# Two weight sums of the first dense unit move within GpSimd's queue, past a key decay and a query decay

## The chip, the cores and the metric

The kernel runs on one core of a Trainium2 chip. The metric is the device time of one execution in microseconds. Of the kernel before there are three timed runs, 581.52, 581.63 and 581.82 us.

## The reference, cut to what matters

```python
# q, k, v: batch 2, heads 8, sequence 768, head size 64, float32
state = gamma * state + outer(k[t], v[t])          # one 64x64 state for each batch and head
y[t]  = scale * q[t] @ state                       # decaying linear attention
x = y as (1536, 512)
h = x @ w_in;  x = (h * sigmoid(1.702 * h)) @ w_out          # dense layer 1, 512 -> 2048 -> 512
xn = x / rms(x) * rms_g
x = (silu(xn @ w_gate) * (xn @ w_val)) @ w_out               # dense layer 2, 512 -> 1536 -> 512
```

## The kernel before

**Attention.** The sequence of each of the 2 batches is cut into 6 chunks of 128 tokens: 12 chunks a = 0 to 11, where 0 to 5 are the first batch. Each engine has one queue, in the order in which its program is written, and works through the chunks in passes of two (`for a in range(0, STEPS, 2)`). For a chunk TensorE does the scores (L396), the products of decayed keys and values that are added to the state ("new products", L413), the part of the output that comes from the state ("from state", L428) and the part from the chunk itself ("from chunk", L441). VectorE masks the scores (L891) and copies or decays the state out of PSUM ("new state", L903 and L906). GpSimd multiplies the keys by their decay ("key decay", `decay_k`, L1039) and, from chunk 7 on, the queries by theirs ("query decay", `decay_q`, L1047). Chunks 5 and 11, the last of each batch, need no key decay and no new products; chunks 0 and 6 need no query decay. ScalarE copies the outputs to SBUF (L694).

In a pass a TensorE's order is: scores of both chunks, from state of both, new products of a + 1, from chunk of both, new products of a + 2. A chunk's new products wait for its key decay and for the new state of the step before; its from-state product waits for its query decay and the same state.

**The first dense unit.** The dense layers multiply blocks in the scheme of Strassen and Winograd, with seven products in place of eight, and each float32 operand is split in a high and a low half that TensorE reads as fp32r. A unit of weights is one transfer to `raw`. GpSimd makes four sums of its blocks (`weight_sum(r, k)`, k = 0 to 3, at L1054, L1057, L1060 and L1064), ScalarE makes the high halves (L605) and VectorE the low halves (L773). In the same way x is summed by VectorE (L795, L796, L799, L803), and split by ScalarE (L624) and VectorE (L782). The sums and splits of unit 0 and of the first batch's x are written between the attention passes, so that TensorE can go from the last from-chunk product straight to the first dense product (L479 to L482). SyncE issues the transfer of unit 0's weights at 16.39 us, behind the key and value transfers of chunks 5 and 6.

VectorE's order around the change, with the chunk or block in brackets: masked (4, 5), low half x (B11, B21), new state (6; the table names it by the chunk that it takes in), masked (6, 7), new state (7), x sums at L795 and L796, low half of weights L773, new state (8), masked (8, 9), low half x (T1), new state (9), low half x (B22), low half of weights, new state (10), masked (10, 11), and the remaining sums and halves.

**GpSimd's order**, by passes, before:

| pass a | order in the queue |
|---|---|
| 2 | key decay 3, key decay 4 |
| 4 | weight sum 0, key decay 6, weight sum 1 |
| 6 | query decay 7, key decay 7, weight sum 2, key decay 8, weight sum 3 |
| 8 | query decays 8 and 9, key decays 9 and 10 |
| 10 | query decays 10 and 11 |

Weight sum 0 waits for the transfer of `raw`; sum 1 waits for sum 0, sum 2 for sum 1, sum 3 for sum 0.

Of the kernel before, what the change touches and what calls it, by code (L numbers as in the profile page):

```python
# [61 lines left out]
def transformer_kernel(nc, attn_in, tables, ident_in, gain_in, w1, w2, out):  # L62
    with ExitStack() as ctx:
# [112 lines left out]
        for p, (layer, _) in enumerate(PHASES):  # L176
            units += [("hidden", p, j) for j in range(HIDDEN[layer])]
            units += [("project", p, j) for j in range(PROJECT[layer])]
# [74 lines left out]
        def cols(i, size):  # L253
            return slice(i * size, i * size + size)
# [39 lines left out]
        def state_at(a):  # L294

            g, c = chunk_of(a)
            return (CHUNKS - 1) * g + min(c, CHUNKS - 1)

        def cross_at(a):

            g, c = chunk_of(a)
            return (CHUNKS - 1) * g + max(c - 1, 0)
# [6 lines left out]
        def set_growth(engine, c):  # L309
            for h in range(HEADS):  # L310
                ins = engine.memset(k_growth[:, HEADS * c + h:HEADS * c + h + 1], HEAD_DIM ** 0.5 * gamma(h) ** (-CHUNK * c))
            return ins
# [70 lines left out]
        def _(pe):  # L383
# [202 lines left out]
            for p, (layer, _) in enumerate(PHASES):  # L586
                for j in range(HIDDEN[layer]):
                    hidden(p, j)
                    if p in (1, 2) and j == 4:
                        norm_totals(p - 1)  # L590
                    if p in (1, 2) and j == 6:
                        norm_bcast(p - 1)
                project_phase(p)

        @block.scalar
        def _(act):
# [117 lines left out]


            for p, (layer, _) in enumerate(PHASES):
                for j in range(HIDDEN[layer]):
                    n, r = h_at[p, j], at["hidden", p, j]
# [307 lines left out]
        @block.gpsimd  # L1026
        def _(pool):
            for c in range(LEAVES):
                ins = set_growth(pool, c)
            ins.then_inc(factors_set, 1)  # L1030
            pool.memset(minus_half[:, :], -0.5).then_inc(half_set, 1)

            def decay_k(a):
                r, m = a % SLOTS, state_at(a)
                pool.wait_ge(kv_in[r], 16 * (a // SLOTS) + 16)
                if m >= 2:
                    pool.wait_ge(kv_done, m - 1)
                k, kd = (t.rearrange("p (h d) -> p h d", h=HEADS) for t in (slot[r][:, 1024:1536], k_dec[m % 2]))
                pool.tensor_tensor(kd, k, k_table[:, cols(a % CHUNKS, HEADS)].unsqueeze(2).to_broadcast([P, HEADS, HEAD_DIM]),  # L1039
                                   ALU.mult).then_inc(k_decayed, 1)  # L1040

            def decay_q(a):
                r, x = a % SLOTS, cross_at(a)
                pool.wait_ge(qk_in[r], 16 * (a // SLOTS) + 16)
                if x >= 2:
                    pool.wait_ge(cross_done, x - 1)
                pool.tensor_tensor(q_dec[x % 2], slot[r][:, 0:512], q_table, ALU.mult)\  # L1047
                    .then_inc(q_decayed[1], 1)

            def weight_sum(r, k):  # L1050
                s1, a11, a12, a21, a22, s2, s4 = (raw[r % 2][:, cols(k, 256)] for k in range(7))
                if k == 0:
                    pool.wait_ge(raw_in[r % 2], 16 * (r // 2) + 16)
                    pool.tensor_tensor(s1, a21, a22, ALU.add).then_inc(w_sums, 1)  # L1054
                elif k == 1:
                    pool.wait_ge(w_sums, sums_at[r] + 1)
                    pool.tensor_tensor(s2, s1, a11, ALU.subtract).then_inc(w_sums, 1)  # L1057
                elif k == 2:
                    pool.wait_ge(w_sums, sums_at[r] + 2)
                    pool.tensor_tensor(s4, a12, s2, ALU.subtract).then_inc(w_sums, 1)  # L1060
                else:

                    pool.wait_ge(w_sums, sums_at[r] + 1)
                    pool.tensor_tensor(a21, a11, a21, ALU.subtract).then_inc(w_sums, 1)  # L1064

            pool.wait_ge(k_table_set, 1)
            decay_k(0)
            for a in range(0, STEPS, 2):
                for b in (a, a + 1):
                    if b > CHUNKS:  # L1070
                        decay_q(b)
                if (a + 1) % CHUNKS < CHUNKS - 1:
                    decay_k(a + 1)
                if a in (4, 6):
                    weight_sum(0, a - 4)
                if a + 2 < STEPS:
                    decay_k(a + 2)
                if a in (4, 6):
                    weight_sum(0, a - 3)

            for r, (kind, p, j) in enumerate(units):
                if kind == "hidden":
                    if r == 1:

                        pool.wait_ge(x_lo_done, 6)
                    for k in range(4):
                        if r > 0:
                            weight_sum(r, k)
                    if p in (1, 2) and j == 6:
                        pool.wait_ge(half_set, 1)  # L1090
                        pool.wait_ge(mean_done, p)
                        pool.tensor_tensor(inv_rms[:, :], mean_sq[:, :], minus_half[:, :], ALU.pow)\
                            .then_inc(inv_done, 1)
# [56 lines left out]
```

## Time and profile before

| | us |
|---|---|
| median of three runs | 581.63 |
| profiled execution, own time | 581.93 |
| its span | 580.1 |
| TensorE busy | 572.4 (99%) |
| VectorE busy | 360.9 (62%) |
| ScalarE busy | 297.8 (51%) |
| GpSimd busy | 170.4 (29%) |

The span is the part of the execution that the profile shows, from its first instruction to its last. The execution's own time is 1.83 us more. An engine's busy time counts its instructions alone; what it waits for stands as idle time before the next instruction. In the rows below PE is TensorE, DVE VectorE, ACT ScalarE and POOL GpSimd. The slot buffers, the decayed keys and queries, the state and the masked scores all lie in one tensor and have the name `arena`.

### The profile page before, as it was taken

Reading aid. Unit: us, or ns where it says so; the run is one execution under the profiler, and the core shown is the slowest. Engines: PE = TensorE matmul, PEld = TensorE weight load, DVE = VectorE, ACT = ScalarE, POOL = GpSimd, SP = SyncE. Lnnn points to the kernel's source line nnn. Section 1 sums busy time; section 2 is a strip of 40 time slices with the busy share of each in tenths; the row PEclk is TensorE's granted clock in tenths of the full one; section 3 lists DMA queues with packets and bytes.
Section 4 is the critical chain, followed back from the end, with each engine's and each line's share of the span. In section 5 each row is a group of like instructions: output and inputs, shape, how many; then the busy total and the mean of one; then the engine's idle time right before and its main releaser. Section 6 shows DMA issues by size and latency. Waiting matters only on the chain.

```text
span 580.1 us, 9395 instructions
## 1 busy us (share of the span) xinstructions
PE 572.4 (99%) x3638; PEld 551.0 (95%) x3638; DVE 360.9 (62%) x486; ACT 297.8 (51%) x501; POOL 170.4 (29%) x222
## 2 busy tenths in 40 slices
PE   7999999999999999999999999999999999999997
PEld 7989999999999999999999999998889999998886
DVE  5899555666325667776336778668755666666432
ACT  1244766654326767544237655574435555564321
POOL 2395643000223461000315454400051545420000
PEclk8999999999999999999999999999999999999999
DMA  8971222322102222312202222232214222224202
GB/s 319 403 284 37 74 72 73 110 72 75 52 21 73 73 72 74 110 41 68 73 0 76 72 73 73 74 101 82 74 36 139 79 73 73 73 74 115 67 1 108
DMA packets 24220, 52.84 MB, mean 91 GB/s; under 512 B 1776, under 2 KB 1904, under 8 KB 24176
## 3 DMA queue, kind: packets, MB, share of 16 engines
q1 hardware_dynamic: 23312, 49.36, 25.6%
q10 hardware_dynamic: 864, 2.88, 1.3%
q8 instruction: 29, 0.48, 0.3%
q14 instruction: 15, 0.12, 0.1%
HBM read 49.09 MB, written 3.15 MB: 90 GB/s over the span
## 4 chain that ended last, share of the span: by engine, by line
PE 93%; DMA 3%; issue 2%; POOL 1%; ACTq 0%; DVE 0%; POOLq 0%
PE bank L532 20%; PE twin L532 20%; PE twin L479 11%; PE twin L482 11%; PE twin L481 11%; PE bank L482 6%; PE bank L481 6%; PE bank L479 6%; DMA arena<-attn_in 3%; PE bank L441 1%; PE bank L428 1%; PE bank L573 0%; POOL arena L1047 0%; PE twin L396 0%; ACTq L684 0%
## 5 line engine op out<-in xcount | busy, mean ns | idle before, releaser
L773 DVE TENSOR_TENSOR w_lo<-raw,w_hi 128x512 fp32r<-128x512 f32 (+2 forms) x148 | 148.9, 1022 | 49.9 <-ACT w_hi L605 49.5
L1054 POOL TENSOR_TENSOR raw<-raw 128x256 f32<-128x256 f32 x40 | 31.4, 786 | 323.3 <-DMA raw<-w 316.5
L479 PE MATMUL twin<-x_hi,w_hi 128*128 128x384 f32 x360 | 120.6, 335 | 0.0
L482 PE MATMUL twin<-x_hi,w_lo 128*128 128x384 f32 x360 | 120.3, 334 | 0.0
L481 PE MATMUL twin<-x_lo,w_hi 128*128 128x384 f32 x360 | 120.3, 334 | 0.0
L605 ACT ACTIVATE w_hi<-raw 128x512 fp32r<-128x512 f32 (+2 forms) x148 | 109.0, 762 | 19.7 <-PE bank L532 7.6
L808 DVE TENSOR_TENSOR g_lo<-arena,g_hi 128x768 fp32r<-128x768 f32 x56 | 54.5, 973 | 75.2 <-ACT g_hi L635 75.2
L635 ACT ACTIVATE g_hi<-arena 128x768 fp32r<-128x768 f32 x56 | 47.4, 847 | 103.8 <-PE bank L532 103.8
L479 PEld LDWEIGHTS twin<-x_hi,w_hi 128*128 128x128 f32 x360 | 67.6, 188 | 0.2 <-issue 0.2
L481 PEld LDWEIGHTS twin<-x_lo,w_hi 128*128 128x128 f32 x360 | 67.6, 188 | 0.0
L482 PEld LDWEIGHTS twin<-x_hi,w_lo 128*128 128x128 f32 x360 | 67.6, 188 | 0.0
L479 PE MATMUL bank<-x_hi,w_hi 128*128 128x384 f32 x200 | 66.9, 334 | 0.0
L481 PE MATMUL bank<-x_lo,w_hi 128*128 128x384 f32 x200 | 66.8, 334 | 0.0
L482 PE MATMUL bank<-x_hi,w_lo 128*128 128x384 f32 x200 | 66.8, 334 | 0.0
L1064 POOL TENSOR_TENSOR raw<-raw 128x256 f32<-128x256 f32 x40 | 45.4, 1136 | 0.0
L532 PE MATMUL twin<-g_hi,w_hi 128*128 128x384 f32 x128 | 42.8, 334 | 0.0
L532 PE MATMUL twin<-g_lo,w_hi 128*128 128x384 f32 x128 | 42.8, 334 | 0.0
L532 PE MATMUL twin<-g_hi,w_lo 128*128 128x384 f32 x128 | 42.8, 334 | 0.0
L532 PE MATMUL bank<-g_lo,w_hi 128*128 128x384 f32 x128 | 42.8, 334 | 0.0
L532 PE MATMUL bank<-g_hi,w_hi 128*128 128x384 f32 x128 | 42.8, 334 | 0.0
L532 PE MATMUL bank<-g_hi,w_lo 128*128 128x384 f32 x128 | 42.8, 334 | 0.0
L1060 POOL TENSOR_TENSOR raw<-raw 128x256 f32<-128x256 f32 x40 | 38.0, 951 | 3.1
(99 smaller groups left out, 997.8 us busy)
## 6 DMA issues: line engine op xcount, KB each, us to landing
raw<-w SPq DMA_DIRECT2D x68, 512.0 KB, 3.4
arena<-attn_in SPq DMA_DIRECT2D x20, 512.0 KB, 9.0
arena<-attn_in ACTq DMA_DIRECT2D x4, 512.0 KB, 12.7
out<-x SPq DMA_DIRECT2D x1, 1536.0 KB, 8.6
out<-x SPq DMA_DIRECT2D x6, 256.0 KB, 2.0
arena<-tables ACTq DMA_DIRECT2D x1, 512.0 KB, 6.1
arena<-tables ACTq DMA_DIRECT2D x1, 256.0 KB, 9.8
ident<-ident_in SPq DMA_DIRECT2D x1, 64.0 KB, 8.5
```

Source lines behind the costliest of these rows:

```text
L428: mm = pe.matmul(gate[par][rows, cols(p, P)], state[x % 2][rows, cols(p, 64)], q_dec[x % 2][rows, cols(p, P)], start=p == 0, stop=False, s ...
L479: pe.matmul(dst, w_hi[q][:, w], x_hi[:, x], start=start and kk == 0, stop=False, skip_group_check=True)
L481: pe.matmul(dst, w_hi[q][:, w], x_lo[:, x], start=False, stop=False, skip_group_check=True)
L482: mm = pe.matmul(dst, w_lo[q][:, w], x_hi[:, x], start=False, stop=kk == 1, skip_group_check=True)
L532: mm = pe.matmul(dst, a, x, start=f == 0 and k == 0, stop=f == TILES[layer] - 1 and k == 2, skip_group_check=True)
L605: act.activation(w_hi[q % 3][:, dst], src, ACT.Copy).then_inc(w_hi_done, 1)
L635: act.activation(g_hi[ft % 3][:, :], g32[:, cols(f, SEQ)], ACT.Copy).then_inc(g_hi_done, 1)
L773: dve.tensor_tensor(w_lo[q % 3][:, dst], src, w_hi[q % 3][:, dst].bitcast(F32), ALU.subtract)\
L808: dve.tensor_tensor(g_lo[ft % 3][:, :], g32[:, cols(f, SEQ)], g_hi[ft % 3][:, :].bitcast(F32), ALU.subtract).then_inc(g_lo_done, 1)
L1054: pool.tensor_tensor(s1, a21, a22, ALU.add).then_inc(w_sums, 1)
L1060: pool.tensor_tensor(s4, a12, s2, ALU.subtract).then_inc(w_sums, 1)
L1064: pool.tensor_tensor(a21, a11, a21, ALU.subtract).then_inc(w_sums, 1)
```

## The change

The order of GpSimd's queue in passes 2 to 6. The number of instructions, their operands and their waits stay as they are, and no other engine's program is touched. After the change pass 2 is key decay 3, key decay 4, weight sum 0, weight sum 1; pass 4 is key decay 6, weight sum 2, weight sum 3; pass 6 is query decay 7, key decay 7, key decay 8. As one line:

```
before: k4 | w0 k6 w1 | q7 k7 w2 k8 w3 | q8 q9 k9 k10 | q10 q11
after:  k4 w0 w1 | k6 w2 w3 | q7 k7 k8 | q8 q9 k9 k10 | q10 q11
```

```diff
                 if (a + 1) % CHUNKS < CHUNKS - 1:
                     decay_k(a + 1)
-                if a in (4, 6):
-                    weight_sum(0, a - 4)
                 if a + 2 < STEPS:
                     decay_k(a + 2)
-                if a in (4, 6):
-                    weight_sum(0, a - 3)
+                if a in (2, 4):
+                    weight_sum(0, a - 2)
+                    weight_sum(0, a - 1)
```

## Rows read from the trace of the kernel before

**Rows 1.** The page's busy times and shares of the span, with instructions.
```profile
PE 572.4 (99%) x3638; PEld 551.0 (95%) x3638; DVE 360.9 (62%) x486; ACT 297.8 (51%) x501; POOL 170.4 (29%) x222
```

**Rows 2.** Windows: length; busy of PE, PEld, DVE, ACT, POOL; PEclk, DMA, GB/s.
```profile
50.10:570.00 519.90, 519.90 (x2885) 504.03 (x2884) 319.47 (x412) 282.62 (x478) 144.28 (x158) 1.00 0.22 71
```

**Rows 3.** Timeline of PE: start, length, instructions, idle before them and its releaser.
```profile
25.44 1.96 PE L428 MATMUL bank<-arena 64*64 64x128 f32 x32
...
29.41 0.69 PE L413 MATMUL bank<-arena 128*64 128x64 f32 x16
...
33.18 0.69 PE L413 MATMUL bank<-arena 128*64 128x64 f32 x16
...
38.05 1.09 PE L428 MATMUL bank<-arena 64*64 64x128 f32 x16
40.00 1.09 PE L428 MATMUL bank<-arena 64*64 64x128 f32 x16 [0.86 <-POOL arena L1047]
...
41.54 1.92 PE L441 MATMUL bank<-arena 128*64 128x128 f32 x32
43.28 0.63 PE L413 MATMUL bank<-arena 128*64 128x64 f32 x16
...
45.83 2.08 PE L428 MATMUL bank<-arena 64*64 64x128 f32 x32
47.86 2.32 PE L441 MATMUL bank<-arena 128*64 128x128 f32 x32
```

**Rows 4.** Timeline of POOL around the four weight sums.
```profile
26.82 0.72 POOL L1054 TENSOR_TENSOR raw<-raw 128x256 f32<-128x256 f32 x1 [5.93 <-DMA raw<-w]
27.50 1.76 POOL L1039 TENSOR_TENSOR arena<-arena 128x512 f32<-128x512 f32 x1
29.22 1.44 POOL L1057 TENSOR_TENSOR raw<-raw 128x256 f32<-128x256 f32 x1
30.63 1.27 POOL L1047 TENSOR_TENSOR arena<-arena 128x512 f32<-128x512 f32 x1
...
33.56 1.03 POOL L1039 TENSOR_TENSOR arena<-arena 128x512 f32<-128x512 f32 x1
34.56 1.44 POOL L1064 TENSOR_TENSOR raw<-raw 128x256 f32<-128x256 f32 x1
35.96 3.94 POOL L1047 TENSOR_TENSOR arena<-arena 128x512 f32<-128x512 f32 x2
39.86 2.04 POOL L1039 TENSOR_TENSOR arena<-arena 128x512 f32<-128x512 f32 x2
```

**Rows 5.** Timeline of DVE in the same stretch.
```profile
26.94 3.14 DVE L782 TENSOR_TENSOR x_lo<-x,x_hi 128x768 fp32r<-128x768 f32 x2
...
31.23 2.36 DVE L891 TENSOR_TENSOR arena<-twin,arena 128x1024 f32<-128x1024 f32 x2 [0.68 <-PE twin L396]
33.91 0.42 DVE L906 TENSOR_TENSOR arena<-bank,arena 128x256 f32<-128x256 f32 x1 [0.33 <-PE bank L413]
34.25 1.16 DVE L795 TENSOR_TENSOR t<-x 128x768 f32<-128x768 f32 x1
35.33 1.48 DVE L796 TENSOR_TENSOR x<-x 128x768 f32<-128x768 f32 x1
36.74 2.03 DVE L773 TENSOR_TENSOR w_lo<-raw,w_hi 128x768 fp32r<-128x768 f32 x1
38.69 0.41 DVE L906 TENSOR_TENSOR arena<-bank,arena 128x256 f32<-128x256 f32 x1
39.02 2.34 DVE L891 TENSOR_TENSOR arena<-twin,arena 128x1024 f32<-128x1024 f32 x2
41.28 1.43 DVE L782 TENSOR_TENSOR x_lo<-x,x_hi 128x768 fp32r<-128x768 f32 x1
42.64 0.41 DVE L906 TENSOR_TENSOR arena<-bank,arena 128x256 f32<-128x256 f32 x1
```

**Rows 6.** Key and value transfer of chunk 9, issued at 28.47: issue to landing.
```profile
DMA to landing us min/median/max: 7.4/7.4/7.4
```

## The prediction

> **What bounds the kernel now.** I read the page's busy times first: TensorE is busy 99% of the span [rows 1]. The windows then say where it has room: from 50.10 to 570.00 it is busy for all of 519.90 us [rows 2]. So there is no slack behind the attention stage, and whatever moves the first dense product (50.11) moves the end by as much. Before that point the timelines of three engines have to be laid side by side.
>
> TensorE [rows 3] has one named wait behind the weights' arrival: from state of chunk 9 starts at 40.00 after 0.86 us idle, released by GpSimd's query decay. A smaller one has no label: new products of chunk 6 start at 29.41, and key decay 6 ends at 27.50 + 1.76 = 29.26 [rows 4], so they follow it at 0.15 us. GpSimd [rows 4] waits 5.93 us for the weights until 26.82 and has no idle time from there to the end of its query decays. VectorE [rows 5] waits 0.33 us for TensorE at 33.91 (new state 7), and from there each of its rows starts where the one before ends. So from 33.91 on VectorE too passes a delay on.
>
> **How GpSimd and VectorE meet.** Rows 4 and 5, side by side, show a pattern. When both have an instruction whose two inputs are in SBUF, the recorded ends alternate at fixed distances: key decay 8 ends at 34.59, the sum at L795 at 35.41, weight sum 3 at 36.00, the sum at L796 at 36.81, and, past the first query decay, the low half at L773 at 38.77 and query decay 9 at 39.90. The held-up VectorE instruction of 768 elements ends 0.82 after GpSimd's, a held-up weight sum 0.59 after VectorE's, a held-up query decay 1.13 after. At the start the same: weight sum 0 ends at 27.54, so the first L782 at 28.36, key decay 6 at 29.26 (0.90 behind it), the second L782 at 30.08 and weight sum 1 at 30.66. Masking (L891) and new state (L906) read one input from PSUM; key decays 9 and 10 beside the masking take 2.04 for two, as key decay 8 alone takes 1.03. Those don't meet. Free durations are therefore: weight sum 0.72, key decay 1.03, query decay 1.27 [rows 4]; consecutive starts overlap by 0.03 to 0.08.
>
> The Trainium skill, SBUF — State Buffer, "Who interferes with whom", states this as an exclusive lock: the one that starts first keeps the shared port for the whole instruction, and the other blocks. By the distances above the trace agrees. If the two only shared bandwidth, the recorded lengths would travel with their instructions, and the sum would be the 1.3 us of the second rival below in place of my 1.9.
>
> **The change, part by part.** Nothing is added or removed; 4 instructions move.
>
> *Weight sum 0* keeps its place (behind key decay 4) and its wait: it ends at 27.54. Price 0.
>
> *Weight sum 1 ahead of key decay 6.* Sum 1 waits for the first L782: 28.36 + 0.59 = 28.95. The second L782 ends 28.95 + 0.82 = 29.77. Key decay 6 ends 29.77 + 0.90 = 30.67, in place of 29.26: +1.41. New products 6 move from 29.41 to 30.82, and in TensorE's queue the scores of 6 and 7 stand behind them, with all that follows. Bounds of this step: +0.69 (a free sum, start to start) and +1.44 (the recorded sum 1).
>
> *Weight sums 2 and 3 ahead of query decay 7.* From 30.67 VectorE holds only masking and new state, so these are free: sum 2 to 31.36, sum 3 to 32.05 (in the kernel before sum 3 met L795 and took 1.44), query decay 7 to 33.29, key decay 7 to 34.29, key decay 8 to 35.29. TensorE, 1.4 late from new products 6, reaches from state 7 at about 33.5 and new products 7 at 34.55 (33.18 before). All three decays are then ready: these two moves cost nothing beyond the 1.4, which already covers them. Were that cover gone, query decay 7 alone would be 33.29 - 31.90 = 1.39 late.
>
> *What meets next.* VectorE's new state 7 follows new products 7 and moves from 33.91 to 35.29, L795 from 34.25 to 35.63. But GpSimd is now ahead: query decay 8 starts at 35.26, before L795. It ends at 36.53; then L795 37.35, query decay 9 at 38.48 (1.4 sooner than before), L796 at 39.30, key decay 9 at 39.30 + 0.90 = 40.20, and L773 at 41.02, where it ended at 38.77. Key decay 9 can take that turn: its keys left at 28.47 and landed 7.4 later, at 35.9 [rows 6], and it needs new products 7. New state 8 starts 2.25 late, at 40.94, and ends at 41.35. From state 9 needs it, so it starts at about 41.5 in place of 40.00: +1.5. The 0.86 us that waited for GpSimd is replaced by a wait of about 1.0 for VectorE (from state 8 would end at 39.14 + 1.4 = 40.5).
>
> *The second meeting.* Masking 8 and 9 move by 2.25, to 41.27 and 43.61. GpSimd: key decay 10 is held up by L773 to 41.92 (41.90 before), query decay 10 is free beside the masking, to 43.15, and query decay 11 starts at 43.12; from state 9, for which it waits, ends at 42.6. L782 (block T1) would start at 41.28 + 2.25 = 43.53, finds query decay 11 ahead, which ends at 44.39, and ends at 45.21 in place of 42.71. New state 9 ends at 45.54; new products 10 need it and start at 45.69 in place of 43.28: +2.4.
>
> *What is given back.* Behind new products 10 TensorE now has no further wait: the from-state pair follows 45.83 - 43.28 = 2.55 later, at 48.2, and the from-chunk pair about 1.9 behind that, at 50.1; the two maskings (2.34) have been running since about 47.4, when scores 10 were done, and end at 49.8. In the kernel before this stretch had hidden waits for VectorE: the pair of from-chunk groups at 47.86 took 2.32, the one at 41.54 took 1.92, and the pair of from-state groups at 45.83 took 2.08 against 1.96 at 25.44 [rows 3]. Given back: 0.40 + 0.12 = 0.52.
>
> **Sum:** 2.4 - 0.52 = +1.9 us on the first dense product, and on the end. The profiled execution took 581.93 (span 580.1 and 1.83 around it) and would take 583.8; it lies 0.30 above the median. Against the median: 581.63 + 1.9 = 583.5.
>
> What the weight sums feed gains nothing: ScalarE's conversions of the parts from sums 2 and 3 stand behind its conversion of L796's result, which ended at 36.81, and sum 3 ended at 36.00 already [rows 4, 5].
>
> **Rivals.**
>
> 1. *Only the first meeting goes as worked out* (query decay 11 misses L782, or key decay 9 and L773 meet in a milder way). From state 9 is 1.5 late, new products 10 too, and 0.52 is given back: +1.0, 582.6. For it: the second meeting hangs on 0.4 us (43.12 against 43.53). Against it: the distances above hold to 0.01 us.
>
> 2. *The delay is carried and nothing new meets*: new state 7 is 1.4 late, VectorE's queue keeps its recorded lengths to masking 11, and the first dense product is 1.3 late: 582.9. For it: VectorE is full from 33.91. Against it: sum 3 is no longer among the instructions that L796 meets, and query decay 8 starts ahead of L795, so lengths must change.
>
> 3. *VectorE's load falls.* Sum 3 leaves L795 and L796, and TensorE catches up at its 0.86 us wait: 1.4 - 0.86 = +0.5, 582.1. It needs L773 ahead of key decay 9. Against it: key decay 9 arrives at 38.45, 0.8 before L773 can start.
>
> 4. *Faster.* Query decay 9 ends before TensorE comes to it, and the 0.86 us wait goes: up to -0.9, 580.8. It decides only if key decay 6 costs TensorE nothing, that is if its end stays near 29.26; beyond 0.86 us of delay at the scores of 8 and 9 this is a loss. For it: that wait is the only long one, and GpSimd is named as its releaser. Against it: new products 6 already start 0.15 us behind key decay 6, and any weight sum ahead of it costs at least 0.69.
>
> 5. *Worse*: in the shifted order one more instruction of VectorE meets a query decay (1.27 with its start overlap, 1.2) ahead of a state or a mask that TensorE waits for: 1.9 + 1.2 = +3.1, 584.7. Against it: by the working above GpSimd is done at 44.39, and only L782 of block T1 lies beside its last query decay.
>
> **How the numbers follow.** Forecast 0.55, rivals 0.12, 0.08, 0.11, 0.05 and 0.09 in this order. This measurement can tell about 0.2%, 1.16 us, from no change. Slower by more than that: the forecast, rival 5 and about the half of rival 2 that lies above 582.8, 0.55 + 0.09 + 0.05 = 0.69. Faster: half of rival 4 at most, 0.04. Within: 0.27. The range leaves out rivals 3 and 4 and a part of 5: 582.3 to 584.4. The forecast's own range is 583.0 to 584.0: the handover between engines (0.10 to 0.15, three times) and 0.2 for the weights' landing.
>
> **What would show it.** Key decay 6 ending near 30.7 and new products 6 at 30.8; query decay 7 no longer a wait; L773 (the first of 768 elements) ending near 41.0; from state 9 at 41.5, released by new state and not by GpSimd; new products 10 near 45.7; the first L479 at about 52.0; and 519.9 us without idle behind it. It is wrong if L773 ends before 40 (rival 3), if L782 of T1 takes 0.95 and not 1.7 (rival 1), or if new products 6 start before 30.1 (rival 4).

## The result and the profile after

The changed kernel takes 583.74 us (median of 7 runs, 583.50 to 584.15); the kernel before took 581.87 in the 7 runs beside and ahead of them (581.52 to 582.70). The medians differ by 1.87 us. The ratio is worked out from the runs apart from the two medians: 1.0027, which is 1.6 us, with a 95% interval of 1.0018 to 1.0036, which is 1.0 to 2.1 us. The prediction was 1.9 us more, 583.5. In the profiled executions the time went from 581.93 to 583.62 and the span from 580.1 to 581.8.

The page of the changed kernel, busy times, and its windows from the first dense product on (length; busy of PE, PEld, DVE, ACT, POOL; PEclk, DMA, GB/s):

```profile
PE 570.9 (98%) x3638; PEld 549.7 (94%) x3638; DVE 359.0 (62%) x486; ACT 297.9 (51%) x501; POOL 168.5 (29%) x222
```

```profile
52.00:570.00 518.00, 518.00 (x2875) 502.47 (x2875) 317.47 (x411) 281.59 (x476) 143.85 (x158) 1.00 0.22 71
```

VectorE and GpSimd are each busy for 1.9 us less than before, and the kernel is slower all the same: the totals of [rows 1] can't show this change. As in [rows 2], TensorE has no idle time behind the first dense product. That product starts at 51.80 in place of 50.11, 1.69 us later, and this is the whole difference between the two profiled executions (583.62 - 581.93 = 1.69). So everything happens in the attention stage.

GpSimd's timeline after, to lay beside [rows 4] (start, length, instruction, idle before it and its releaser):

```profile
26.57 0.72 POOL L1054 TENSOR_TENSOR raw<-raw 128x256 f32<-128x256 f32 x1 [5.70 <-DMA raw<-w]
27.38 1.33 POOL L1057 TENSOR_TENSOR raw<-raw 128x256 f32<-128x256 f32 x1
28.66 1.76 POOL L1039 TENSOR_TENSOR arena<-arena 128x512 f32<-128x512 f32 x1
30.38 0.73 POOL L1060 TENSOR_TENSOR raw<-raw 128x256 f32<-128x256 f32 x1
31.07 0.72 POOL L1064 TENSOR_TENSOR raw<-raw 128x256 f32<-128x256 f32 x1
31.76 1.27 POOL L1047 TENSOR_TENSOR arena<-arena 128x512 f32<-128x512 f32 x1
32.99 2.03 POOL L1039 TENSOR_TENSOR arena<-arena 128x512 f32<-128x512 f32 x2
34.99 3.22 POOL L1047 TENSOR_TENSOR arena<-arena 128x512 f32<-128x512 f32 x2
38.17 3.47 POOL L1039 TENSOR_TENSOR arena<-arena 128x512 f32<-128x512 f32 x2
41.60 2.51 POOL L1047 TENSOR_TENSOR arena<-arena 128x512 f32<-128x512 f32 x2
```

Key decay 6 ends at 28.66 + 1.76 = 30.42, where it ended at 29.26. But query decays 8 and 9 are now done at 38.21, 1.7 us sooner than before: what TensorE waited for at 40.00 comes early.

VectorE's timeline after, to lay beside [rows 5]:

```profile
35.03 0.42 DVE L906 TENSOR_TENSOR arena<-bank,arena 128x256 f32<-128x256 f32 x1 [0.29 <-PE bank L413]
35.37 1.71 DVE L795 TENSOR_TENSOR t<-x 128x768 f32<-128x768 f32 x1
37.00 2.02 DVE L796 TENSOR_TENSOR x<-x 128x768 f32<-128x768 f32 x1
38.94 1.79 DVE L773 TENSOR_TENSOR w_lo<-raw,w_hi 128x768 fp32r<-128x768 f32 x1
40.66 0.41 DVE L906 TENSOR_TENSOR arena<-bank,arena 128x256 f32<-128x256 f32 x1
40.99 2.34 DVE L891 TENSOR_TENSOR arena<-twin,arena 128x1024 f32<-128x1024 f32 x2
43.25 1.67 DVE L782 TENSOR_TENSOR x_lo<-x,x_hi 128x768 fp32r<-128x768 f32 x1
44.85 0.41 DVE L906 TENSOR_TENSOR arena<-bank,arena 128x256 f32<-128x256 f32 x1
```

Look at the four long rows. L795, L796, L773 and L782 have one shape (128x768). L795 takes 0.95 when nothing holds it up (the last experiment); here the four take 1.71, 2.02, 1.79 and 1.67, 7.19 in all. In [rows 5] the same four took 6.10. Other rows of VectorE are shorter than before, which is how its total can fall: the pair of L782 ahead of this stretch takes 2.61 in place of 3.14, and the L782 and the L773 behind it take 0.94 and 0.68 in place of 1.70 and 1.75.

TensorE's timeline after, to lay beside [rows 3]:

```profile
30.57 0.69 PE L413 MATMUL bank<-arena 128*64 128x64 f32 x16 [1.29 <-POOL arena L1039]
...
39.11 1.09 PE L428 MATMUL bank<-arena 64*64 64x128 f32 x16
41.22 1.09 PE L428 MATMUL bank<-arena 64*64 64x128 f32 x16 [1.01 <-DVE arena L906]
...
45.41 0.69 PE L413 MATMUL bank<-arena 128*64 128x64 f32 x16 [0.73 <-DVE arena L906]
...
48.01 1.97 PE L428 MATMUL bank<-arena 64*64 64x128 f32 x32
49.90 1.97 PE L441 MATMUL bank<-arena 128*64 128x128 f32 x32
51.80 0.44 PE L479 MATMUL twin<-x_hi,w_hi 128*128 128x384 f32 x1
```

One wait of 0.86 us for GpSimd has become three: 1.29 for key decay 6, 1.01 and 0.73 for VectorE's new states 8 and 9. The chain of work that ended last, followed back from 52 to 36 us in the changed kernel, names who holds the end up (start, length, what; only its part up to new products 10 is shown, and TensorE's own work follows). In the kernel before the chain from 36 to 51 us had the query decays (14.3% of it) and TensorE in it, and no instruction of VectorE:

```profile
35.37 1.71 DVE t L795
37.08 1.94 DVE x L796
39.02 1.26 DVE w_lo L773
40.28 0.38 issue
40.66 0.41 DVE arena L906
41.07 1.94 DVE arena L891 x2
43.01 0.25 issue
43.25 1.67 DVE x_lo L782
44.92 0.35 DVE arena L906
45.27 0.14 issue
45.41 0.69 PE bank L413 x16
```

### The profile page after: what moved, and what is told of

It is laid out like the page before. It is cut to its first block, busy times and chain, and to the rows that moved or that the text cites. A ratio compares the mean times of both kernels' runs of the same rounds, so it can differ in the third digit from the quotient of the medians.

```text
span 581.8 us, 9395 instructions
## 1 busy us (share of the span) xinstructions
PE 570.9 (98%) x3638; PEld 549.7 (94%) x3638; DVE 359.0 (62%) x486; ACT 297.9 (51%) x501; POOL 168.5 (29%) x222
## 4 chain that ended last, share of the span: by engine, by line
PE 93%; DMA 3%; DVE 2%; POOL 1%; issue 0%; ACTq 0%; SPq 0%; DVEq 0%; POOLq 0%
PE bank L532 20%; PE twin L532 20%; PE twin L479 11%; PE twin L481 11%; PE twin L482 11%; PE bank L481 6%; PE bank L479 6%; PE bank L482 6%; DMA raw<-w 2%; DMA arena<-tables 2%; PE bank L428 1%; PE twin L396 1%; PE bank L441 0%; PE bank L413 0%; PE bank L573 0%; DVE x L796 0%
## 5 line engine op out<-in xcount | busy, mean ns | idle before, releaser
L773 DVE TENSOR_TENSOR w_lo<-raw,w_hi 128x512 fp32r<-128x512 f32 (+2 forms) x148 | 147.4, 1012 | 49.2 <-ACT w_hi L605 49.0
```

What stands on the lines that cost most here:

```text
L773: dve.tensor_tensor(w_lo[q % 3][:, dst], src, w_hi[q % 3][:, dst].bitcast(F32), ALU.subtract)\
```

## The experiments

The theory: a GpSimd instruction that reads SBUF and a VectorE instruction with two SBUF inputs take turns, each held up for the whole of the other, and the order in which they come up sets the time of this stage. Such a hold-up is called a meeting below. Every number expected below was worked out from the rows above with the same distances as the prediction (0.82 behind a GpSimd instruction; 0.59, 0.90 and 1.13 behind a VectorE instruction). In the diffs `w` is a weight sum of unit 0, `k` a key decay, `q` a query decay, and the line is GpSimd's queue from the first weight sum on. "Later" and "earlier" are against the median of the kernel before in the same comparison: 581.93 for the first four, 582.08 for the next four, 581.78 for the last four. The changed kernel was timed in its own comparison alone, so what is said against its 583.74 is uncertain by the 0.3 us by which the medians of the kernel before differ.

**Sum 1 alone.** Against the kernel before:

```diff
-w0 k6 w1 q7 k7 w2 k8 w3 q8 q9 ...
+w0 w1 k6 q7 k7 w2 k8 w3 q8 q9 ...
```

> Only weight sum 1 is moved, ahead of key decay 6; sums 2 and 3 stay where the kernel before has them. Theory (GpSimd and VectorE alternate through an exclusive lock, and the order of meetings decides): key decay 6 ends near 30.6 instead of 29.26, new products 6 start near 30.7. GpSimd's work ahead of query decay 8 is the same as in the changed kernel, so that decay starts at 35.1, before L795, and both waits for VectorE's new state come back: from state 9 at 41.3 and new products 10 at 45.5. The end is 1.9 us later than before, as with the whole change. Rival (a delay that is merely carried, with no new meetings): 1.3 us later. Rival (each moved sum costs its own share): clearly less than the whole change, 0.7 to 1.2 us.

Measured: 583.80, 1.87 later, ratio 1.0030 (1.0018 to 1.0041). New products 6 start at 30.69, query decay 8 at 35.12, from state 9 at 41.34, new products 10 at 45.52. The first of the three moved sums gives the whole loss. The interval (1.0 to 2.4 us) would leave room for a delay merely carried (1.3) and for the upper end of a price for each instruction (0.7 to 1.2); the trace doesn't, as both waits for VectorE's new state are in it (1.12 us at from state 9, 0.73 at new products 10).

**Sums 2 and 3 alone.** Against the kernel before:

```diff
-w0 k6 w1 q7 k7 w2 k8 w3 q8 q9 ...
+w0 k6 w1 w2 w3 q7 k7 k8 q8 q9 ...
```

> Only weight sums 2 and 3 are moved, ahead of query decay 7; sum 1 stays behind key decay 6. Theory of the lock: new products 6 stay near 29.3, query decay 7 ends at 33.3 instead of 31.90 and holds TensorE there instead; new state 7 is 1.3 us late all the same, query decay 8 starts before L795, and from state 9 (41.4) and new products 10 (45.6) wait for VectorE. The end is 1.9 to 2.1 us later than before. The rival that each moved sum costs its own share: what the run with sum 1 alone leaves of the 1.9, 0.7 to 1.2 us. That neither sum 2 nor 3 matters, as the prediction priced them at nothing behind the delay of sum 1: within 0.3 us of before.

Measured: 583.93, 2.00 later (ratio 1.0033, 1.0020 to 1.0045). The two moves that the prediction priced at nothing cost as much as the whole change when they are made alone; behind sum 1's delay they cost nothing more. One expected number missed: in the profiled execution VectorE came to its low halves 0.3 us sooner and met weight sum 0 (1.29 in place of 0.72), so new products 6 started at 30.00 and not near 29.3. Weight sum 1 then met nobody (0.73 in place of 1.44), which gave the time back: query decay 7 ended at 33.26 (33.3 expected), TensorE waited 0.85 us for it, and from state 9 started at 41.45, new products 10 at 45.64. That the later instants came as expected owes something to these two cancelling.

**Key decay 6 first.** Against the changed kernel:

```diff
-w0 w1 k6 w2 w3 q7 k7 k8 q8 q9 ...
+k6 w0 w1 w2 w3 q7 k7 k8 q8 q9 ...
```

> The changed kernel with key decay 6 ahead of weight sum 0 (queue: key 6, sums 0 to 3, query 7, key 7, key 8, ...). Key decay 6 then runs near 24.9 while GpSimd waits for the weights, and new products 6 start at 29.1. Theory of the lock: query decay 7 ends near 32.2 and new state 7 is only 0.2 to 0.3 us later than before, but query decay 8 starts (34.1) before L795 (34.4), so L796 and L773 are each held up by one decay more: from state 9 at 40.35, released by new state 8, new products 10 at 44.5, and the end is 1.0 us later than before and 0.9 earlier than the changed kernel. Rival of the carried delay: with hardly a delay left to carry, the end is no later than before (0 to 0.3 us earlier, since query decay 9 is ready sooner and the wait of 0.86 us goes).

Measured: 582.68, 0.75 later than before (ratio 1.0011, 1.0002 to 1.0020) and 1.06 earlier than the changed kernel's 583.74, with ranges that don't overlap (582.45 to 583.06 against 583.50 to 584.15). The 1.0 expected against before lies inside the interval. This run sets the meetings apart from the delay. GpSimd and TensorE:

```profile
33.96 3.22 POOL L1047 TENSOR_TENSOR arena<-arena 128x512 f32<-128x512 f32 x2
```

```profile
28.91 0.64 PE L413 MATMUL bank<-arena 128*64 128x64 f32 x16
...
40.19 1.09 PE L428 MATMUL bank<-arena 64*64 64x128 f32 x16 [1.01 <-DVE arena L906]
...
44.38 0.69 PE L413 MATMUL bank<-arena 128*64 128x64 f32 x16 [0.73 <-DVE arena L906]
```

New products 6 are 0.5 us *sooner* than in the kernel before, query decays 8 and 9 are done at 37.2, and the kernel is still slower, since query decay 8 (33.96) came up ahead of L795 (34.35). TensorE waited 0.73 us for query decay 7, but new state 7, at 34.01, is only 0.10 later than in the kernel before: next to nothing is left to carry. The waits of 1.01 and 0.73 are those of the changed kernel, to the hundredth.

**Without the second meeting.** Against the changed kernel, in VectorE's pass 8:

```diff
-                elif a == 8:
-                    lower_x(0, T1)
                 new_state(a + 1)
+                if a == 8:
+                    lower_x(0, T1)
```

> The changed kernel, and in VectorE's queue the low half of block T1 (L782) stands behind new state 9 instead of ahead of it. This takes away the second meeting alone. Theory of the lock: from state 9 still waits for new state 8 (41.3), but new state 9 starts right behind masking 9 near 43.4, new products 10 at 44.5 instead of 45.4 without an idle time before them; the end is 0.9 us earlier than the changed kernel, 1.0 us later than before. Rival (VectorE is simply full, so that order within it does not matter): the end stays within 0.2 us of the changed kernel, masking 11 ending as late as there.

Measured: 582.91, 0.98 later than before (ratio 1.0013, 1.0004 to 1.0022), 0.83 earlier than the changed kernel. From state 9 waits 1.01 us for new state 8 as ever, new products 10 start at 44.69 with no idle time ahead of them, and the first dense product starts at 51.03. VectorE does the same work in another order. The move takes more away from new state 9 than the hold-up of L782, which was 1.67 - 0.95 = 0.72: L782's own 0.95 goes as well. The run shows that L782 in that place costs 0.83 us; it doesn't price the meeting by itself.

**Without the first meeting.** Against the changed kernel, in VectorE's queue:

```diff
+                if a == 8:
+                    lower_w(0, 0)
                 masked(a + 1)
 ...
                     sum_x(0, T1)
-                    lower_w(0, 0)
```

> The changed kernel, and in VectorE's queue the low half of the first weights (L773, 768 elements) stands behind masking 8 instead of ahead of new state 8. This takes the first meeting off new state 8. Theory of the lock: L796 is still held up to 39.2 by query decay 9, new state 8 starts at 39.1 instead of 40.66, from state 9 starts at 40.2 without a wait; the low half meets key decay 10 or none, L782 of T1 is free, new products 10 start near 44.3. The end is 1.2 us earlier than the changed kernel, 0.8 later than before. Rival (only the 1.3 us delay of new products 6 counts, not the meetings): the end stays within 0.3 us of the changed kernel.

Measured: 582.75, 0.67 later than before (ratio 1.0012, 1.0003 to 1.0021), 0.99 earlier than the changed kernel. Against the kernel before of each comparison the gain is 1.87 - 0.67 = 1.20, and 1.2 was expected. From state 8 and 9 run as one pair; new products 10 start at 44.58, after 0.20 us. Here too the instruction's own 0.95 leaves the way of new state 8 together with its hold-up of 1.79 - 0.95 = 0.84. In its new place L773 takes 1.33, and L782 of block T1 takes 0.94: the second meeting goes with the first.

**The kernel before with key decay 6 first.**

```diff
-w0 k6 w1 q7 k7 w2 k8 w3 q8 q9 ...
+k6 w0 w1 q7 k7 w2 k8 w3 q8 q9 ...
```

> The kernel before with key decay 6 ahead of weight sum 0, and sum 1 then directly behind sum 0 (queue: key 6, sums 0 and 1, query 7, key 7, sum 2, key 8, sum 3, query 8, ...). Theory of the lock: new products 6 start at 29.1 and not 29.41; sum 3 is done near 34.2, query decay 8 starts at 34.1, behind L795 (33.8) as in the kernel before, so the meetings keep their order; from state 9 starts at 39.4 instead of 40.0. Part of it is lost again at new products 10, which wait for new state 9. The end is 0.25 us earlier than before, 0.1 to 0.5. Rival of the first wait alone (what is won at 40.00 is won at the end): 0.65 us earlier.

Measured: 581.83, 0.25 earlier, which the interval doesn't tell from nothing (ratio 0.9996, 0.9988 to 1.0005). Its trace shows the mechanism: from state 9 at 39.51, now released by new state 8 after 0.75 us, and new products 10 at 43.46 after 0.50 us. What is won at the first wait turns into a wait for VectorE.

**Two orders made from the theory.** Both against the kernel before; the first has VectorE's `lower_x(0, T1)` behind new state 9 as well.

```diff
-w0 k6 w1 q7 k7 w2 k8 w3 q8 q9 k9 k10 q10 q11
+k6 w0 w1 q7 w2 k7 k8 w3 q8 q9 k9 k10 q10 q11
```

> Made from the theory of the lock to beat the kernel before. GpSimd: key 6, sums 0 and 1, query 7, sum 2, key 7, key 8, sum 3, query 8 and on; VectorE: low half of T1 behind new state 9. Query decay 8 (34.1) stays behind L795 (33.8); new state 9 starts right behind masking 9 at 41.4, so new products 10 start at 42.6 instead of 43.28, and from chunk 11 waits for masking 11 near 48. Theory of the lock: the first dense product 0.85 us earlier than in the kernel before, 0.5 to 1.0. Rival (masking 11, at the end of VectorE's full queue, sets it): 0.3 us earlier or less.

```diff
-w0 k6 w1 q7 k7 w2 k8 w3 q8 q9 k9 k10 q10 q11
+k6 w0 q7 k7 k8 q8 w1 w2 q9 k9 k10 w3 q10 q11
```

> Only GpSimd's queue differs from the kernel before: key 6, sum 0, query 7, key 7, key 8, query 8, sums 1 and 2, query 9, key 9, key 10, sum 3, query 10 and 11. All decays that TensorE waits for stand ahead of the sums that are not due. Theory of the lock: new products 6 at 29.1, new state 7 at 33.5, L773 ends near 38.0 (38.77 before), from state 9 at 39.2, new products 10 at 42.5; the first dense product 0.85 us earlier, 0.4 to 1.0, as the sums then needed by ScalarE (sum 2 by 37.1, sum 3 by 42.4) come in time. Against it: sum 2 and sum 3 end close to where ScalarE asks for them, and ScalarE's outputs of chunks 8 and 9 stand behind its halves of the weights; if they hold up from state 10, the end is as late as before or later.

Measured: 581.21, 0.87 earlier (ratio 0.9988, 0.9979 to 0.9996), and 581.04, 1.04 earlier (ratio 0.9983, 0.9974 to 0.9991), where 0.5 to 1.0 and 0.4 to 1.0 were expected. In the profiled executions new products 10 start later than expected, at 42.99 (42.6) and 43.29 (42.5); the last section comes back to the second. In the second all four sums stand *later* than in the kernel before: the opposite of the change, with the opposite sign. Key decay 6 ahead of the first of them gives 0.25 of it, by the run before.

**An x sum in VectorE's gap.** GpSimd's queue and one move on VectorE, against the kernel before; L795 is the first half of `sum_x(0, T1)`, which has a third argument for it here.

```diff
-w0 k6 w1 q7 k7 w2 k8 w3 q8 q9 k9 k10 q10 q11
+k6 w0 w1 q7 k7 k8 q8 w2 q9 k9 w3 k10 q10 q11
```

```diff
-                    sum_x(0, T1)
+                    sum_x(0, T1, 2)      # the rest
 ...
                 if a + 2 < STEPS:
                     new_state(a + 2)
+                if a == 4:
+                    sum_x(0, T1, 1)      # t3 = b22 - b12 alone
```

> Made from the theory of the lock to beat the kernel before. GpSimd's queue: key 6, sums 0 and 1, query 7, key 7, key 8, query 8, sum 2, query 9, key 9, sum 3, key 10, query 10 and 11. VectorE: the first x sum (L795) stands behind new state 6, in the 0.7 us in which VectorE waited for scores 6, instead of behind new state 7. Theory of the lock: L795 ends near 31.6, L796 near 35.5, L773 near 37.0 (38.77 before), from state 9 and new products 10 start without any wait at 38.6 and 41.9, and the first dense product is 1.7 us earlier than in the kernel before, 1.2 to 1.8. Rival (the 0.86 us wait at 40.00 is all that TensorE can win in this stage): 0.9 us earlier.

Measured: 579.98 (579.76 to 580.20), 1.80 earlier than the kernel before, ratio 0.9963 (0.9951 to 0.9976), and 3.8 earlier than the changed kernel. It beats both. TensorE and, behind it, VectorE (in this kernel L891 has become L894 and the first x sum L796):

```profile
37.23 1.96 PE L428 MATMUL bank<-arena 64*64 64x128 f32 x32
39.12 0.69 PE L413 MATMUL bank<-arena 128*64 128x64 f32 x16
41.38 0.67 PE L413 MATMUL bank<-arena 128*64 128x64 f32 x16
...
47.91 0.44 PE L479 MATMUL twin<-x_hi,w_hi 128*128 128x384 f32 x1
```

```profile
29.86 1.49 DVE L796 TENSOR_TENSOR t<-x 128x768 f32<-128x768 f32 x1
31.28 2.34 DVE L894 TENSOR_TENSOR arena<-twin,arena 128x1024 f32<-128x1024 f32 x2
```

From state 8 and 9 are one pair without a wait, and new products 10 have none either. The bound of 0.9 us that the rival set is passed, by as much again: L796 now runs in VectorE's idle time ahead of the masking.

**The same move alone**, on the kernel before and on the changed kernel:

> The kernel before with only L795 moved behind new state 6; GpSimd's queue as before. Theory of the lock: L795 starts at 30.4 and is then done by 31.4, but query decay 7 meets it and ends at 32.5 instead of 31.90, so from state 7 starts at 32.65; L796 ends 36.0, L773 37.4, query decay 9 at 39.8 as before and from state 9 at 39.9; new products 10 at 43.2. Masking 11 ends at 47.6 instead of 48.9, so the stall of 0.5 us behind new products 10 goes: the end is 0.35 us earlier than before, 0.1 to 0.6. Rival (VectorE's full queue is the bound, and it gets 1.2 us of room): 1.0 us earlier.

> The changed kernel with only L795 moved behind new state 6. It takes the first of the three VectorE instructions out of the stretch where they alternate with query decays 8 and 9 and key decay 9. Theory of the lock: new products 6 stay at 30.7, query decay 7 meets L795 and ends at 33.9, new state 7 is 0.7 us later than in the changed kernel, but new state 8 starts at 39.8 instead of 40.7 and from state 9 has no wait (40.9); L782 of T1 no longer finds query decay 11 ahead and new products 10 start at 44.3 instead of 45.5. The end is 1.2 us earlier than the changed kernel and 0.7 later than before, 0.4 to 1.0. Rival (the late key decay 6 alone makes the 1.9 us): no more than 0.3 us earlier than the changed kernel.

Measured: 581.33, 0.45 earlier than before (ratio 0.9990, 0.9981 to 0.9999), and 582.50, 0.72 later than before (ratio 1.0008, 0.9999 to 1.0016), which is 1.24 earlier than the changed kernel. In the first the query decay that L795 now meets is what TensorE waits for next (from state 7 at 32.77, 0.79 us idle, released by it), so of the 1.33 us by which masking 11 ends sooner (47.61 in place of 48.94) a third reaches the end. In the second new products 6 are as late as in the changed kernel (30.69 against 30.57) and about two thirds of the loss are gone.

**Which accesses meet.** Against the changed kernel:

```diff
-                pool.tensor_tensor(q_dec[x % 2], slot[r][:, 0:512], q_table, ALU.mult)\
-                    .then_inc(q_decayed[1], 1)
+                ins = (pool.memset(q_dec[x % 2], 0.5) if a in (8, 9) else
+                       pool.tensor_tensor(q_dec[x % 2], slot[r][:, 0:512], q_table, ALU.mult))
+                ins.then_inc(q_decayed[1], 1)
```

> The changed kernel with query decays 8 and 9 on GpSimd replaced by memsets of the same 128x512 outputs: GpSimd then writes them and reads nothing, and the outputs of chunks 8 and 9 are not the reference's. It asks whether it is GpSimd's reading that holds VectorE up. Theory of the lock on the read side: L795 takes 0.95 and L796 takes 0.95 or, if it meets key decay 9, 1.8; L773 ends near 39 instead of 40.7, from state 9 starts without a wait for new state 8 at 40.3, new products 10 at 44.4 or sooner; the end is 0.9 to 1.3 us earlier than the changed kernel. Rival (any GpSimd instruction that touches SBUF holds the port, writing too): L795 and L796 take 1.7 and 2.0 less what the memset is shorter than a decay, and the gain follows that length. The trace of before has memsets of 128x1 alone (0.10), so their length here is open.

Measured: 582.56, 0.78 later than before (ratio 1.0008, 1.0000 to 1.0017). That is 1.09 us less than the changed kernel loses, within the 0.9 to 1.3 that were expected. The kernel leaves out two decays, so its output is not the reference's. GpSimd and VectorE:

```profile
35.22 0.98 POOL L1047 MEMSET arena<- 128x512 f32 x2
36.18 3.01 POOL L1039 TENSOR_TENSOR arena<-arena 128x512 f32<-128x512 f32 x2
```

```profile
35.62 0.95 DVE L795 TENSOR_TENSOR t<-x 128x768 f32<-128x768 f32 x1
36.49 1.80 DVE L796 TENSOR_TENSOR x<-x 128x768 f32<-128x768 f32 x1
```

The two memsets end at 36.20, and L795 runs from 35.62 to 36.57 beside them without a loss on either side. L796, which meets key decay 9, takes 1.80. Each memset takes 0.52, the first half beside new state and the second wholly beside L795. The rival, that any access holds the other up, would have given a longer L795 or a longer second memset. So GpSimd's writing alone doesn't hold VectorE up, and the decays that read do. The memsets are also shorter than the decays (0.98 for two in place of 3.22), so the 1.09 us is not the price of the reading alone; the rows answer the question, not the time.

## Why the prediction was right

It forecast 1.9 us, and the medians differ by 1.87. That the two agree to 0.03 us is closer than the timed runs can tell, whose interval is 1.0 to 2.1 us and has room for rival 2's 1.3; what bears the mechanism out is the instants in the trace. The weights landed 0.25 us sooner in the profiled execution after (26.57 against 26.82), so each predicted instant is to be read 0.25 lower:

| step | predicted, less 0.25 | measured |
|---|---|---|
| key decay 6 ends | 30.42 | 30.42 |
| new products 6 start | 30.57 | 30.57 |
| query decay 7 ends | 33.04 | 33.03 |
| query decay 8 starts, ahead of L795 | 35.01 | 34.99 |
| L773 ends | 40.77 | 40.73 |
| from state 9 starts | 41.25 | 41.22 |
| new products 10 start | 45.44 | 45.41 |
| lag given back behind them | 0.52 | 0.44 |

The last line: from new products 10 to the first dense product the kernel before took 50.11 - 43.28 = 6.83, the changed one 51.80 - 45.41 = 6.39. The term is 0.08 too large in the prediction, mostly because a from-chunk pair takes 1.97 here (at 49.90) and not the 1.92 read at 41.54. Without the earlier landing the profiled executions would, by the same shift, differ by 1.69 + 0.25 = 1.94.

*Sum 1 ahead of key decay 6* was the cause of the delay: shown by the run with sum 1 alone (new products 6 at 30.69) and the two with key decay 6 first. *Sums 2 and 3 at nothing* was right for this change and only there: alone they cost 2.00 (interval 1.2 to 2.6), through query decay 7. The text said that without the cover that decay would be 1.39 late, and it was 1.36 late (33.26 against 31.90); what it left out is that this lag by itself brings the same meetings, so that the first dense product comes 1.92 later (52.03).

*The first meeting* (rival 3 was to be without it): the trace of the changed kernel shows it, and moving L773 out of it gives 0.99 us back. *The second meeting* (rival 1 was to be without it): the trace shows it too, and moving L782 gives 0.83 back. The two can't be added, and neither is the price of the meeting alone: each move also takes 0.95 of work out of the way, and without the first meeting the second goes too, while without the second the first stays (1.01 us at from state 9). *The carried delay* (rival 2, 1.3 us) is refuted by key decay 6 first, which with 0.10 us of delay left at new state 7 still lost 0.75 (interval 0.1 to 1.2), and by the lengths of VectorE's rows, which don't stay as recorded. *Faster* (rival 4) had the right wait and the wrong end: in the run of the kernel before with key decay 6 first GpSimd's decay no longer held TensorE, and 0.25 us came of it, not told from nothing, where up to 0.9 stood open. *Worse* (rival 5) didn't occur: GpSimd was done with its last query decay at 44.1. Two of the shares in the prediction's chances are rounded up (0.05 for about half of 0.08, and 0.04 for at most half of 0.05); nothing hangs on it.

The Trainium skill, SBUF — State Buffer, names the condition as well ("Who interferes with whom": a VectorE instruction with two SBUF inputs contends with a GpSimd instruction that reads SBUF, not with one that only writes it). The run with memsets agrees: 0.95 beside a memset, 1.80 behind a key decay.

## What to carry to other kernels

Where GpSimd and VectorE both work from SBUF, lay their timelines side by side and write down the order in which their instructions come up. A move in one queue that makes no instruction longer can change that order, and the engine that pays may be the other one. Before moving work that is not due forward, ask what stands behind it; here the gain lay in moving it back (1.04 us), and in giving VectorE a job for the time in which it waited anyway.

## What was not expected

The distances hold far more closely than a timed run can tell. Over the fourteen traces, from 24 to 51 us, a held-up VectorE instruction of 768 elements ends 0.81 to 0.82 us behind GpSimd's, a held-up weight sum 0.58 to 0.60 behind VectorE's, a key decay 0.90 to 0.91 and a query decay 1.12 to 1.14. Each is 0.13 to 0.14 less than what the same instruction takes when free (0.95, 0.72, 1.03 and 1.27): nearly all of a held-up instruction's work lies behind the end of the other, which is what "held up for the whole of the other" looks like in the rows. The profiled executions differ more among themselves: weights landed between 26.46 (the fastest kernel) and 27.12, and in the profiles of two runs (T1 behind the state, and the sums late) the masking of chunks 4 and 5 began at 25.62 and 25.67 where the changed kernel has 24.63. In the first of the two weight sum 1 then met nobody (0.73), and new products 6 started at 30.09 and not 30.7; the first dense product still started where it was expected, since new state 7 was as late by then. In the second the profile alone shows no gain (first dense product at 50.20), while the median of eleven timed runs is 1.04 us earlier. That profiled execution is also the slowest of the eleven, 582.05 us against a median of 581.04: of effects of one microsecond at the start of a kernel, a single profile can't give the size.
